# Attention plus two mixing layers on one core: the spatial mix's tail contracts over 128 rows, and the value projection's tail uses one stationary of high and low halves

## The reference

```
attention (8 heads of 64): q_s = softmax(q over the head's 64), k_s = softmax(k over the 576 tokens)
                           x = q_s @ (k_s^T @ v)
first MoE:  h = gelu(x @ w_in)          # 512 -> 1024; u = h[:, :512], v = h[:, 512:]
            v_n = (v - mean) / sqrt(var + 1e-6) * g_ln
            v_s[t] = sum_s w_sg[t, s] * v_n[s] + b_sg[t]      # the spatial mix, over the 576 tokens
            x1 = x + (u * v_s) @ w_out
second MoE: h = relu(x1 @ w_in2); conv of 3 taps over the tokens; out = (h * sigmoid(conv)) @ w_out2
```

## Time and profile before

| what | us |
|---|---|
| three runs | 1013.30, 1016.92, 1018.04 (median 1016.92) |
| profiled execution, span from first to last instruction | 1014.0 |
| TensorE busy (matmuls) | 972.6 (96%) |
| VectorE busy | 665.1 (66%) |
| ScalarE busy | 408.9 (40%) |
| GpSimd busy | 358.6 (35%) |
| mean granted TensorE clock | 0.990 of full |
| matmuls at line 375 (value projection) | 480, busy 117.4 |
| matmuls at line 505 (the mix's tail) | 128, busy 30.5 (16.8 of it over 64 rows) |

### The profile page before, as it was taken

How to read it: one execution, slowest core, us unless ns; L and a number is a source line. 1 busy time by engine, 2 the same in 40 slices (tenths; PEclk the granted TensorE clock), 3 DMA queues, 4 the chain that set the end, 5 groups by cost and what they waited for, 6 DMA issues and landing times.

```text
span 1014.0 us, 17663 instructions
## 1 busy us (share of the span) xinstructions
PE 972.6 (96%) x6816; PEld 933.1 (92%) x6816; DVE 665.1 (66%) x992; ACT 408.9 (40%) x656; POOL 358.6 (35%) x241
## 2 busy tenths in 40 slices
PE   3779999999999999999999998999999999999998
PEld 2669989999899999998999897999999999999998
DVE  8894783865856838748645678675757575757560
ACT  5454352543544434534422444343434343434331
POOL 4455264353352542634421413322222232323230
PEclk9989999999999999999999998999999999999999
DMA  7511403113104022031020241002020202020001
GB/s 252 156 53 26 157 22 122 50 31 114 57 21 137 34 83 98 26 119 57 21 82 27 89 162 47 25 20 76 12 83 13 83 12 81 12 81 12 36 19 52
DMA packets 32395, 67.40 MB, mean 66 GB/s; under 512 B 2912, under 2 KB 2912, under 8 KB 32352
## 3 DMA queue, kind: packets, MB, share of 16 engines
q1 hardware_dynamic: 27744, 57.37, 17.2%
q10 hardware_dynamic: 4608, 9.44, 2.4%
HBM read 46.87 MB, written 18.87 MB: 65 GB/s over the span
## 4 chain that ended last, share of the span: by engine, by line
PE 80%; DVE 14%; issue 3%; ACT 2%; DMA 1%; POOL 0%; DVEq 0%; SPq 0%; ACTq 0%
PE psum L383 64%; PE psum L375 8%; DVE plain_arena L1101 3%; PE psum L505 2%; DVE plain_arena L1076 2%; PE psum L431 2%; PE psum L400 2%; PE psum L412 1%; DVE plain_arena L1005 1%; DVE split_arena L1035 1%; PE psum L433 1%; ACT plain_arena L737 1%; DMA plain_arena<-in_q 1%; DVE plain_arena L1028 1%; DVE plain_arena L994 1%
## 5 line engine op out<-in xcount | busy, mean ns | idle before, releaser
L383 PE MATMUL psum<-split_arena 128*128 128x288 f32 x5568 | 764.0, 298 | 9.9 <-DVE split_arena L1139 5.2
L383 PEld LDWEIGHTS psum<-split_arena 128*128 128x128 f32 x5568 | 750.4, 190 | 16.8 <-issue 7.4
L1438 POOL TENSOR_TENSOR plain_arena<-plain_arena 128x576 f32<-128x576 f32 x64 | 107.3, 1677 | 295.3 <-ACT plain_arena L913 295.3
L375 PE MATMUL psum<-split_arena 128*128 128x512 f32 x480 | 117.4, 397 | 0.1
L1281 DVE TENSOR_SCALAR plain_arena<-plain_arena 128x576 f32<-128x576 f32 x64 | 39.9, 623 | 114.1 <-ACT plain_arena L907 114.1
L375 PEld LDWEIGHTS psum<-split_arena 128*128 128x128 f32 x480 | 89.7, 191 | 17.8 <-DVE split_arena L1062 0.4
L1286 DVE SCALAR_TENSOR_TENSOR plain_arena<-plain_arena 128x576 f32<-128x576 f32 x64 | 96.9, 1514 | 2.3
L907 ACT ACTIVATE plain_arena<-psum 128x576 f32<-128x576 f32 x64 | 41.5, 650 | 93.2 <-PE psum L383 58.7
L1349 POOL TENSOR_TENSOR split_arena<-plain_arena,split_arena 128x512 fp32r<-128x512 f32 (+1 forms) x40 | 51.4, 1286 | 75.8 <-ACT split_arena L687 75.8
L1337 POOL TENSOR_TENSOR plain_arena<-plain_arena 128x1024 f32<-128x1024 f32 (+1 forms) x24 | 39.0, 1636 | 98.6 <-DVE plain_arena L994 98.6
L1121 DVE TENSOR_TENSOR split_arena<-plain_arena,split_arena 128x576 fp32r<-128x576 f32 x32 | 24.3, 759 | 68.6 <-ACT split_arena L759 68.4
(11 more groups left out here) (71 smaller groups left out, 959.3 us busy)
## 6 DMA issues: line engine op xcount, KB each, us to landing
x_dram<-plain_arena ACTq DMA_DIRECT2D x32, 288.0 KB, 2.1
plain_arena<-x_dram SPq DMA_DIRECT2D x8, 1152.0 KB, 5.6
outT<-plain_arena SPq DMA_DIRECT2D x32, 288.0 KB, 2.1
plain_arena<-in_v SPq DMA_DIRECT2D x32, 256.0 KB, 4.2
plain_arena<-in_kT SPq DMA_DIRECT2D x7, 1152.0 KB, 8.4
plain_arena<-in_q SPq DMA_DIRECT2D x7, 1024.0 KB, 5.6
plain_arena<-in_w_in SPq DMA_DIRECT2D x8, 512.0 KB, 4.9
plain_arena<-in_w_out SPq DMA_DIRECT2D x6, 512.0 KB, 4.5
```

What stands on the lines that cost most here:

```text
L375: mm = e.matmul(out, stat[s], mov[m], start=first and n == 0, stop=last and n == 2, skip_group_check=True)
L383: mm = e.matmul(out[:, h, 0:NH], stat[s], mov[m][:, h * NH:(h + 1) * NH], start=first and n == 0, stop=last and n == 2, skip_group_check=True)
L1438: e.tensor_tensor(gt[:, f % 2, :], gt[:, f % 2, :], hp[:, f % 2, 1:T + 1], ALU.mult).then_inc(hg_full, 1)
```

## The change

It has two parts.

**The mix's tail.** Both matmuls now contract over 128 rows, so the second also adds low by low. Their count and columns stay.

**The value projection's tail.** The tail's columns of x are copied into a new stationary `x_tail`: the 64 high columns by ScalarE (`hi_x_tail`), the 64 low ones beside them by VectorE (`lo_x_tail`). Per block d two matmuls (by the high and by the low weights) replace three. Output rows 0 to 63 hold the high part and rows 64 to 127 the low part. ScalarE copies the latter down (`copy_tail`), VectorE adds them (`sum_tail`), and the gelu reads the sum. The tail's matmuls all stand behind block 3 of the other units now. `x_tail` uses the place of `gT`.

```diff
@@ tensor: v_part
+                    if u == 2:
+                        if d == 0:
+                            e.wait_ge(x_tail_hi, b + 1)
+                            e.wait_ge(x_tail_lo, b + 1)
+                        for m in (0, 1):
+                            mm = e.matmul(tail_bank, x_tail[:, d, :], win[m][:, d, F:2 * F],
+                                          start=d == 0 and m == 0, stop=d == DT - 1 and m == 1,
+                                          skip_group_check=True)
+                        continue
@@ tensor: sg_unit
-                    for rows, m in ((P, 0), (TAIL, 1)):
+                    for m in (0, 1):
                         for h in HALVES:
-                            mm = e.matmul(main_sets[f % 2][:, h, 0:NH], vn[0][0:rows, j, cols],
-                                          wsg[m][0:rows, j, h * NH:(h + 1) * NH], start=False, stop=m == 1,
+                            mm = e.matmul(main_sets[f % 2][:, h, 0:NH], vn[0][:, j, cols],
+                                          wsg[m][:, j, h * NH:(h + 1) * NH], start=False, stop=m == 1,
@@ tensor: body
-                v_part(m, 2, [0, 1])
                 late = isinstance(m, int) and m == 0
                 ...
-                v_part(m, 2, [DT - 2, DT - 1])
+                v_part(m, 2, list(range(DT)))
@@ scalar
+            def hi_x_tail(b):
+                if not (isinstance(b, int) and b == 0):
+                    e.wait_ge(o_done, b * DT)
+                e.wait_ge(x_hi, b * DT + DT)
+                e.activation(x_tail[:, :, 0:TAIL], xT[0][:, :, TF:T], ACT.Identity).then_inc(x_tail_hi, 1)
@@ scalar: gelu_v
+                if u == 2:
+                    e.wait_ge(v_tail_sum, b + 1)
+                src = vg[0:rows, t:t + n, :] if u == 2 else main_sets[u]
@@ scalar
+            def copy_tail(b):
+                e.wait_ge(v_done, b * NU + NU)
+                e.activation(vg[0:TAIL, NJ - 1, :], tail_bank[TAIL:P, :], ACT.Identity).then_inc(v_tail_lo, 1)
@@ scalar: body
                 hi_x(m, DT - 1)
+                hi_x_tail(m)
                 ...
                 gelu_v(m, 0)
                 gelu_v(m, 1)
+                copy_tail(m)
                 tile(0)
                 gelu_v(m, 2)
@@ vector
+            def lo_x_tail(b):
+                if not (isinstance(b, int) and b == 0):
+                    e.wait_ge(o_done, b * DT)
+                e.wait_ge(x_lo, b * DT + DT)
+                e.tensor_copy(x_tail[:, :, TAIL:P], xT[1][:, :, TF:T]).then_inc(x_tail_lo, 1)
+            def sum_tail(b):
+                e.wait_ge(v_tail_lo, b + 1)
+                place = vg[0:TAIL, NJ - 1, :]
+                e.tensor_tensor(place, tail_bank[0:TAIL, :], place, ALU.add).then_inc(v_tail_sum, 1)
@@ vector: body
                 lo_x(m, DT - 1)
+                lo_x_tail(m)
                 ...
                 moments(m, 0)
                 tile(0)
+                sum_tail(m)
                 moments(m, 1)
```

More of the change, by code:

```diff
@@ L133, in build @@
         tail_bank = psum[:, 4, :]
+        x_tail = split_arena[:, G_AT:G_AT + DT * P].rearrange("p (d n) -> p d n", d=DT)
         kv_sums = psum[:, 4:6, :].rearrange("p a (b h n) -> p (a b) h n", b=2, h=2)
@@ L177, in build @@
             sem(n) for n in ("v_done", "v_gelu", "v_ready", "v_var", "v_rstd", "vn_full", "vn_hi", "vn_lo"))
-        vn_tail = sem("vn_tail")
+        x_tail_hi, x_tail_lo = sem("x_tail_hi"), sem("x_tail_lo")
+        vn_tail, v_tail_lo, v_tail_sum = sem("vn_tail"), sem("v_tail_lo"), sem("v_tail_sum")
         ln_chain, v_sums = sem("ln_chain"), sem("v_sums")
@@ L462, in v_part @@
                             e.wait_ge(w_lo, d + 1)
+                    if u == 2:
[7 more added lines that the diff above has]
+                        continue
                     for n, j in enumerate(UNITS[u]):
-                        out = tail_bank if u == 2 else main_sets[u][:, n, :]
+                        out = main_sets[u][:, n, :]
                         at = d * T + j * P
@@ L735, in gelu_v @@
                     e.wait_ge(w_sg_lo[1], 1)
-                src = tail_bank[0:rows, :].unsqueeze(1) if u == 2 else main_sets[u]
+                if u == 2:
+                    e.wait_ge(v_tail_sum, b + 1)
+                src = vg[0:rows, t:t + n, :] if u == 2 else main_sets[u]
                 e.activation(vg[0:rows, t:t + n, :], src, ACT.Gelu_apprx_tanh).then_inc(v_gelu, 1)
+            def copy_tail(b):
+                e.wait_ge(v_done, b * NU + NU)
+                e.activation(vg[0:TAIL, NJ - 1, :], tail_bank[TAIL:P, :], ACT.Identity).then_inc(v_tail_lo, 1)
             def hi_vn(b, u):
@@ L981, in _ @@
             e.memset(ks[:, DT * T:DT * T + P - TAIL], 0.0).then_inc(pad_set, 1)
-            e.memset(f32(split_arena[:, G_AT:G_AT + P - TAIL]), 0.0).then_inc(pad_set, 1)
             for h in HALVES:
```

## The result

| | kernel before | kernel after |
|---|---|---|
| median of all runs, us | 1016.35 (1013.3 to 1018.04, 4 runs) | 1025.8 (1024.27 to 1026.57, 4 runs) |
| profiled execution: span, us | 1014.0 | 1022.5 |
| granted TensorE clock, mean | 0.990 | 0.983 |
| ratio after/before | | 1.0096, 95% interval 1.0077 to 1.0115 |

The forecast was 1018.8 with a range of 1009 to 1029. The time lies in the range, but the sum behind it was +1.9 us and the measured difference is +9.45. The outcome that had the largest chance, no measurable change, is not what happened.

The account below looks back on a forecast made before the run. TensorE, busy 96% of the span, was taken as the bound. Bodies 1 to 6 at +0.62 each (1.69 - 1.07), +3.7, body 7 -1.7 and body 0 -0.1 gave +1.9 on 1016.92: 1018.8 us, range 1009 to 1029.

Parts of the forecast that it names:

- rival 1: lo_x_tail loses the port to lo_v(a, 0); VectorE's delay is 2.61 instead of 1.69 us; 1024.3 us, chance 0.22.
- rival 3: Mix's tail: the change brings nothing, the 0.19 to 0.39 us at line 505 stay; 1027.9 us, chance 0.07.
- the two meeting places: Body's transposes at 340.17 and 356.71: TensorE waits 0.18 us for GpSimd's scale_q(a, 0), 0.47 for VectorE's lo_k(a, 1).
- The tail's first six matmuls bring nothing: Ahead of the transposes: TensorE idles 1.47 us until scale_q(a, 0) ends, and block 3 starts at 340.58 as before.
- VectorE's delay of 1.69 at `turn_k(a, 2)`: copy_tail and sum_tail delay VectorE's row, moving turn_k(a, 2) from 356.71 to 358.40, 1.69 us per body.
- `lo_x_tail` at the boundary, nothing added: VectorE's lo_x_tail slips in ahead of lo_v(a, 0); moments(m, 0) starts near 344.2, ends before 346.54, adding nothing.
- The mix's tail, 1.07 per body: Line 505: no more row switching saves 0.34 for units 0 and 1, 0.39 for unit 3; 1.07 us per body.
- Body 7, -1.7 forecast: Last body, without transposes: 0.14 us kept behind sum_tail plus 4 x 0.39 of the mix, -1.7 us.
- Body 0, -0.1 forecast: First body: +1.5 at kv_piece(1, 0), less 0.57, less 1.07; about -0.1, 1 us either side for the clock.
- rival 2: All bodies: only TensorE's work counts and neither wait costs anything; 16.3 us gained, 1000.6 us, chance 0.08.
- rival 4: At the transposes: VectorE's instructions run closer, delay about 1.0 instead of 1.69 us; 1014.7 us, chance 0.14.
- rival 5: Added idle in every body brings the clock down, 3 us more in each of six bodies; 1037 us, chance 0.04.

Follow-up runs that it names:

- experiment 5: Kernel after with 16 extra identity transposes on TensorE at the start, nothing else changed; 1019.93 us, ratio 1.0038.
- experiment 8: Kernel before with the mix's tail over 128 rows and lo_k(a, 1), lo_q(a, 1) ahead of normalise(m, 1); 1003.2 us, ratio 0.9865.
- experiment 3: Kernel after with ScalarE's copy_tail behind hi_k(a, 0) and hi_q(a, 0) instead of ahead of them; 1023.95 us, ratio 1.0086.
- experiment 4: Kernel after with VectorE's lo_k(a, 1) and lo_q(a, 1) ahead of normalise(m, 1) and normalise(m, 2); 1020.45 us, ratio 1.0052.
- experiment 1: Kernel before with only the mix's tail changed, to 128 rows; 1007.27 us, ratio 0.989.
- experiment 2: Kernel after with the mix's tail back over 128 and 64 rows, so only the value projection is changed; 1030.15 us, ratio 1.0166.
- experiment 9: Kernel before with 118 identity transposes at its start and nothing else changed; 1023.14 us, ratio 1.008.
- experiment 6: Kernel before with 118 calls of 8-column matmuls on TensorE ahead of its first work, which became 236 matmuls; 1052.51 us, ratio 1.0385.
- experiment 7: Kernel after with tail blocks 0 and 1 ahead of the transposes, all x_tail copies on ScalarE, and the edits of experiments 3, 4 and 5; 1007.77 us.
- experiment 10: Kernel before with 134 identity transposes at its start and nothing else changed; 1017.65 us, ratio 1.0031.

## Why the prediction was right, and where it was short

That the time lies in the range is partly luck. The sum has no term for what experiment 5 takes away with nothing but padding, 5.9 of the 9.45 us; the range was wide for the sake of rivals 1 and 3, which did not come. Padded, the kernel is 4.8 us slower than before (1019.93 against 1015.17) where the sum says 1.9.

- **What bounds the kernel, and the two meeting places:** right. In experiment 8 both waits are gone and the body is the shortest.
- **The tail's first six matmuls bring nothing, because `turn_q(a, 0)` waits for `scale_q(a, 0)`:** right; block 3 starts at the same place in the body. The idle time, 1.48 us from start to start, is split in two, though, so the single wait of 1.4 to 1.5 us that was to show it is not there. `turn_k(a, 0)` waits 0.45 us for `lo_x(m, 3)` (L1086), which I had overlooked: I let TensorE run on at 338.26 without asking when the last low half of x comes. It is hidden behind the later wait and cost nothing.
- **VectorE's delay of 1.69 at `turn_k(a, 2)`:** right in mechanism, 1.81 in size (361.07 - 2.55 - 356.71). `kv_piece(a, 0)` came 1.16 late (352.00 - 2.55 - 348.29) where I had 0.79: 0.15 of the rest is `lo_k(a, 0)`, the others the hand-overs around `sum_tail` and its gelu, which I had made too short. So the wait left at `turn_k(a, 2)` is 1.13 and not 1.4. Experiments 3 and 4 show both links.
- **`lo_x_tail` at the boundary, nothing added:** right on the point that was in doubt. It took 1.42 us with its wait for the port, and `moments(m, 0)` came within 0.1 us of the forecast.
- **The mix's tail, 1.07 per body:** right; 1.03 measured by itself (experiment 1). Rival 3 is out.
- **Sum of a middle body:** 69.3 forecast, 69.39 measured; over six bodies +4.4 against +3.7.
- **Body 7, -1.7 forecast, +1.16 measured:** the step that failed is "so 0.14 is kept, and 4 x 0.39 of the mix". The first half of it held: from the start of the body to the end of the wait for the gelu of u (1.66 us, where the earlier trace rows has 1.00) it is 25.83 us against 26.00, 0.17 kept. The second half did not, since TensorE waits twice more behind it:

```profile
564.81 6.65 PE L386 MATMUL psum<-split_arena 128*128 128x288 f32 x48 [1.66 <-ACT plain_arena L776]
572.19 0.80 PE L517 MATMUL psum<-split_arena 128*128 128x288 f32 x4 [0.72 <-DMA split_arena<-split_arena]
587.36 11.45 PE L386 MATMUL psum<-split_arena 128*128 128x288 f32 x84 [1.59 <-DVE split_arena L1157]
```

  I priced the mix's matmuls of body 7 as if nothing waited after them. The wait at 587.36 is for VectorE's gates, the same that took experiment 1's gain (1.35 us). It is there in experiment 5 too, where the wait at the tail is not:

```profile
584.51 11.45 PE L386 MATMUL psum<-split_arena 128*128 128x288 f32 x84 [1.15 <-DVE split_arena L1159]
```

  Body 7 there takes 58.71, 0.26 less than before: that is what is left of the 1.7. ScalarE, which works for the gates too, waits in that stretch for the weights of the output projection:

```profile
573.29 1.06 ACT L792 ACTIVATE split_arena<-plain_arena 128x1024 fp32r<-128x1024 f32 x1 [4.33 <-DMA plain_arena<-in_w_out]
```

  It does so in the kernel before as well (3.85 us). That this DMA is what sets the floor was read from the rows and not tried. The wait for the DMA at 572.19 goes with the place of the code in part only. It is in after and in experiments 2, 3 and 9 (0.70 to 0.82 us), whose second loop starts at the same place, but not in 4, which starts there too; the kernel before and experiments 1, 5, 6, 7, 8 and 10 do not have it. Body 7 takes 1.42 us more in after than in experiment 5, and 1.96 more in 9 than in 10. What brings this about stays open; an instruction load passes in that stretch in all of them.
- **Body 0, -0.1 forecast, +1.20 measured, 0.3 beyond the 1 us to either side that I gave it.** TensorE ran at a clock of 0.66 between 70 and 80 us (0.83 before), with a wait of 1.33 us in the stretch, which I had priced:

```profile
70.00:80.00 10.00, 7.31 (x35) 7.10 (x36) 9.72 (x30) 3.72 (x6) 4.93 (x5) 0.66 0.01 2
...
73.35 0.55 PE L434 MATMUL psum<-split_arena 128*128 128x256 f32 x1 [1.33 <-ACT plain_arena L756]
```

  The wait does not explain the clock, however. Experiments 2, 3 and 5 have the same wait (1.34 us), the clock in that stretch is 0.83, and body 0 takes 82.41, 81.35 and 81.55; in experiment 4 it is 0.66 again, and 82.96. What decides between the two stays open, and so does whether the placing of the code has a part in it: 2 and 3 have after's.
- **The second MoE: not in the sum at all,** and what happened there is the largest single cost that the sum lacks. (In the table it shows as 2.59 only, less than body 7's miss of 2.9, because of the quicker matmuls behind the stall.) I took code that the change does not touch to cost what it cost. But the change takes 21 TensorE instructions away ahead of it, and with that TensorE loads the loop's code again while it runs: 38 loads for 29, 4.0 us of standing still, the low clock behind it, 6.9 us in all. Experiments 5, 9 and 10 show that this goes and comes with nothing but padding. The step that failed is thus the row that the sum does not have, the second MoE at nothing.
- **Rivals:** 2 and 4 are out. 5 happened in one place, and not the one I named: no wait in a body brought the clock down, but the stop at the loop did; the granted clock of bodies 1 to 6 is 1.00.

**What each part is worth,** then: the mix's part about 8 us faster (experiment 1), the value projection's part 1.83 us per body slower, the placing of the code some 5.5 to 6 us slower (5.9 between after and experiment 5, in which body 0's 1.5 may be chance; 5.5 between 9 and 10, of which 10 has 2.3 us more work ahead of body 0). Even mended and padded, the value projection's part stands behind leaving it out: 67.33 against 66.91 us per body (experiments 7 and 8). Its removed matmuls were what TensorE did while it would have waited, and in their place come a copy and an addition on ScalarE and VectorE, on the path.

## What to carry to other kernels

Ask of each matmul that goes what TensorE would do in its place; ahead of a wait that stays put it is free, and an addition on VectorE that its removal needs may not be. Where a large unchanged loop follows a change, compare the number of instruction loads on the page, and the waits put down to "issue", before the difference is laid on the change. A handful of dummy instructions ahead of the loop, where the engine is idle anyway, tells the two apart in one run (experiment 5); how many instructions they become and how long they take has to be read from the trace (experiment 6).

## What the runs showed of the hardware that I had not expected

**The loop's place in the instruction stream.** Counted in the compiled kernels, the loop of the second MoE has 1575 TensorE instructions, and a load brings 16 KB (0.48 MB in 29). Where it starts, in instructions and modulo 256:

| kernel | start | modulo 256 | loads | stall |
|---|---|---|---|---|
| before | 4819 | 211 | 29 | no |
| after | 4798 | 190 | 38 | yes |
| 5, after with 16 transposes | 4829 | 221 | 29 | no |
| 6, before with 236 small matmuls (counted as in its trace) | 5290 | 170 | 40 | yes |
| 7 | 4834 | 226 | 29 | no |
| 9, before with 118 transposes | 5054 | 190 | 39 | yes |
| 10, before with 134 transposes | 5086 | 222 | 30 | no |

Experiments 1 and 8 start where before does and have no stall; 2, 3 and 4 start where after does and have it. The stall costs 3.3 us (experiment 6) to 6.9 us (after), and 9 makes nine loads more than 10, after nine more than before. The kernels without a stall make no load for some 120 us in the loop's second pass, so the loop is still there; those with it load a block every 16 us or so to the end. The Trainium skill (Runtime: NRT & Kernel Launch, "Instruction fetch mechanics") gives TensorE's buffer as 2048 instructions, filled in blocks of 256. By that page, as an estimate, a loop of 1575 is 6.15 blocks and touches seven or eight of them by its place, which is close to what there is room for. The table agrees in that the place decides, and in the size of a load. But the number of blocks does not sort the kernels: by these starts the loop touches seven at 170, 190 and 211, of which the last has no stall, and eight at 221, 222 and 226, which have none. The page's other rule, that a taken branch to a target outside the current window of two pages has to wait for its fetch, would put a stall at the jump in every kernel; before and experiments 5, 7 and 10 have none. Where exactly between 190 and 211 the edge lies, and by what way the place decides, was not tried.

**64 rows and 128 rows in turn.** In each unit of the mix, two matmuls over 64 rows among others over 128 cost 0.34 to 0.39 us more than two over 128, by the rows of the kernel before; with all of them over 128 rows each body is 1.03 us shorter (experiment 1), though the weights of the two are then twice as high. Nothing was saved here by contracting over fewer rows.

**Two paces of the same matmuls.** The matmuls of the second MoE start every 0.1333 us in nine of the twelve profiled executions, and every 0.1300 in a part of the other three; in after and experiment 2 it changed at the stall, from 0.1333 to 0.1300, and in experiment 6 the other way. In 3, 4 and 9 it did not change at the stall. Over 3072 matmuls this would be 10 us, about as much as single runs fell out of their row (998.19 among some at 1007 in experiment 1, 994.6 among some at 1003 in experiment 8); none of those runs was profiled, so that this is the reason is not shown. What sets the pace is open.

**An fp32 matmul of 8 columns is two.** 118 calls gave 236 matmuls of 0.21 us each (experiment 6), while a transpose of 128 x 128 stays one and took 0.12 to 0.13 (experiments 9 and 10; 0.22 for the 16 of experiment 5).
